# Moving the later weight tiles, and every tile allocated with them, 384 bytes further on in each partition

## The chip, the cores and the metric

The kernel runs on one core of a Trainium2 chip. The metric is the device time of one execution in microseconds. Three executions of the kernel before took 852.66, 852.87 and 853.97 us (median 852.87). An execution that was profiled took 852.58 us; its profile spans 850.8 us from the first to the last instruction.

## The reference

Three parts follow each other. The attention is banded: every query sees the 128 keys up to its own, with a bias that grows with distance. Two feed-forward layers follow, without normalisation or residual between them.

```python
scores = scale * np.matmul(q, k.transpose(0, 1, 3, 2))          # q, k, v: (4, 8, 576, 64)
mask = (rel >= 0) & (rel < window)                              # window = 128
scores = np.where(mask, scores + bias[None], -1000000000.0)
attn = softmax(scores); attn_out = np.matmul(attn, v)
x = attn_out.transpose(0, 2, 1, 3).reshape(B * S, H * D)        # (2304, 512)
h = x @ w_in;  g = h * (1.0 / (1.0 + np.exp(-1.702 * h)));  x = g @ w_out    # 512 -> 2048 -> 512
h = x @ w_in2; g = piecewise square of h, clipped at -1 and 1;  out = g @ w_out2
```

(The softmax is written out in the reference; it is shortened here.)

## The kernel before

**Attention (0 to about 138 us).** Heads are handled in 16 pairs. Queries and keys are split into a high part in fp32r (`qk_hi`) and a remainder (`k_lo`), so that a score is the sum of two fp32r matmuls with 256 columns each (L1009, the first step's L981). The probabilities are transposed on TensorE (L1022), copied, and multiplied with the values (L1043, L1037); the pair's output is transposed once more (L1052, L1057). All tiles of this stage are allocated behind `half`.

**Feed-forward (about 138 to 848 us).** Each layer is done in two phases, so there are four (u = 0 to 3). A phase has an *up* part (its quarter of x @ w_in) and a *down* part (its quarter of g @ w_out), each over three chunks c of 768 tokens. A chunk's product is a 2 x 2 block product done with seven multiplications instead of eight (P1 to P7); the seven combinations of the activations and of the weights are made by VectorE and ScalarE. Each combination is kept as a rounded fp32r value and its remainder, and a product is the sum of three fp32r matmuls for each step along the contraction: weights high x activations high, high x low, low x high. All of this is issued by `multiply` at line L1075.

**Which operand is which.** In all up parts, and in the down parts of phases 0 and 1, the weights are the stationary operand (loaded 128 x 128 by LDWEIGHTS) and the activations in `arena` are the moving one, with 384 columns. In the down parts of phases 2 and 3 ("swapped" below) it is the other way round: the stationary operand is a 128 x 128 block of `arena`, and the moving one is 256 columns of the weights.

**Where the weights lie.** Six slots hold combined weights, slot = w mod 6 for weight pair w. Slots 0 to 2 are the tile `w_first`, slots 3 to 5 the tile `w_rest`:

```python
def w_place(w):
    slot = w % W_SLOTS
    return w_first[:, slot] if slot < 3 else w_rest[:, slot - 3]
```

A phase u uses the pairs 8u to 8u+3 in its up part and 8u+4 to 8u+7 in its down part. So of the four pairs of an up part 1, 3, 2 and 1 lie in `w_rest` in phases 0 to 3. In the down parts, where the four pairs are the four steps of the contraction (in this order), the places are rest, rest, first, first (phase 0); first, first, first, rest (phase 1); first, rest, rest, rest (phase 2); rest, rest, first, first (phase 3).

**Addresses in a partition.** Tiles are allocated one behind the other. The program as compiled has 1152 bytes ahead of the first tile. `before_w_first` and `before_arena` are fillers of 64 bytes, as is `half`, of which one element is used. This gives the starts below; every slot, combination, high or low part and block inside `w_first`, `w_rest` and `arena` is a multiple of 512 bytes further on (`arena`: 1536-byte rows, so too).

| tile | start in bytes | modulo 512 | modulo 256 |
|---|---|---|---|
| `w_first` | 1216 | 192 | 192 |
| `arena` | 44288 | 256 | 0 |
| `half` | 124160 | 256 | 0 |
| `qk_hi` (attention) | 143680 | 320 | 64 |
| `w_rest` | 130368 | 320 | 64 |

The tiles of the attention and those of the feed-forward behind `half` (`d1s`, `w_rest`, `g`, `ust`, `raw_rest`) share the same memory, one set after the other. In `qk_hi` all keys and queries start at multiples of 256 bytes from the tile's start.

**Order.** Each engine's instructions are in an order written out by hand. TensorE runs P1 to P4 of a chunk and waits for `lo_made` (activations ready, from VectorE), for `seeded_b`, `seeded_c` and `d_copied` (ScalarE), and for `c21_out` and `c22_done` (the banks of earlier products read out).

Of the kernel before, what the change touches and what calls it, by code (L numbers as in the profile page):

```python
# [20 lines left out]
F32 = mybir.dt.float32  # L21
# [4 lines left out]
P = 128  # L26
# [86 lines left out]
def build(nc, qkT, v_main, v_tail, w_pairs, bias_table, identity, out):  # L113
# [3 lines left out]
    def sb(name, shape, dt, into=ctx):  # L117
        return into.enter_context(nc.sbuf_tensor(name, shape, dt))
# [17 lines left out]
    arena = sb("arena", [P, ARENA * 4 * HALF], F32R)  # L136
    raw_first = sb("raw_first", [P, 3, 4 * HALF], F32)
    wst = sb("wst", [P, 12, 2 * P], F32)
    half_line = sb("half", [P, 16], F32)
    half = half_line[:, 0:1]  # L140

    qk_raw = sb("qk_raw", [P, SPLIT_RING, WIDTH], F32, attn_ctx)
# [1914 lines left out]
```

## Time and profile before

| | |
|---|---|
| median of three runs | 852.87 us (852.66 to 853.97) |
| profiled execution | 852.58 us, of which the span 850.8 us |
| TensorE matmuls, busy | 843.7 us, 99% of the span |
| VectorE / ScalarE / GpSimd busy | 84% / 63% / 14% |
| mean granted TensorE clock | 0.999 of full |
| first and last matmul of L1075 | 138.4 us and 847.4 us |

In the timeline view a row merges neighbouring instructions of one form: start, length, engine, line, operation, output <- inputs, count. The length runs to the modelled end of the last matmul, which overlaps the next one's start. The time that TensorE needs for a matmul in a stream is therefore taken from the starts of two rows: their distance divided by the number of matmuls between them. In square brackets stands idle time before the row and what ended it.

### The profile page before, as it was taken

How to read it: one execution, taken by the hardware profiler on the slowest of the kernel's cores; microseconds unless marked ns; L12 is line 12 of the kernel's file. 1: busy time of each engine (PE TensorE's matmuls, PEld its weight loads, DVE VectorE, ACT ScalarE, POOL GpSimd, SP SyncE). 2: the span in 40 equal slices, each digit the busy share in tenths (PEclk: the TensorE clock that was granted, in tenths of full speed). 3: DMA queues.
4: the chain of work that ended last, by engine and by line, in shares of the span. 5: the costliest groups of instructions: out<-in, count | busy, mean ns of one | idle time of the engine just before them, and what ended most of it. 6: DMA issues, size and time to landing. Idle time of an engine off the chain costs nothing.

```text
span 850.8 us, 15510 instructions
## 1 busy us (share of the span) xinstructions
PE 843.7 (99%) x5744; PEld 839.7 (99%) x5744; DVE 711.4 (84%) x982; ACT 538.5 (63%) x791; POOL 116.4 (14%) x82
## 2 busy tenths in 40 slices
PE   8999999999999999999999999999999999999998
PEld 8999999999999999999999999999999999999998
DVE  7888898786988966778998987989989788889794
ACT  7778787767775546768644556767555567665441
POOL 3788988000000000000000000000000000000000
PEclk9999999999999999999999999999999999999999
DMA  8888661667676347687764772587647643888822
GB/s 203 226 213 217 191 180 67 268 253 277 250 253 226 133 150 272 250 303 240 260 246 184 287 242 105 210 282 260 235 152 262 231 154 128 291 294 304 310 83 75
DMA packets 63257, 186.45 MB, mean 219 GB/s; under 512 B 7504, under 2 KB 14352, under 8 KB 59344
## 3 DMA queue, kind: packets, MB, share of 16 engines
q1 hardware_dynamic: 62896, 185.30, 63.3%
q8 instruction: 47, 0.77, 0.3%
q14 instruction: 26, 0.21, 0.1%
q10 hardware_dynamic: 288, 0.16, 0.1%
HBM read 113.09 MB, written 72.35 MB: 218 GB/s over the span
## 4 chain that ended last, share of the span: by engine, by line
PE 92%; DVE 5%; POOL 1%; issue 1%; ACT 0%; DVEq 0%; POOLq 0%
PE ps L1075 79%; PE ps L1043 4%; PE ps L1009 3%; PE ps L1022 3%; DVE arena L1755 1%; PE ps L972 1%; POOL qk_hi L895 1%; PE ps L1037 1%; POOL k_lo L892 1%; PE ps L1052 1%; DVE probs L1645 1%; DVE qk_hi L1613 0%; DVE raw_first L1714 0%; DVE g L1787 0%; DVE raw_first L1709 0%
## 5 line engine op out<-in xcount | busy, mean ns | idle before, releaser
L1075 PE MATMUL ps<-arena,w_first 128*128 128x384 f32 x1764 | 328.6, 336 | 0.0
L1075 PEld LDWEIGHTS ps<-arena,w_first 128*128 128x128 f32 x1764 | 307.2, 188 | 0.9 <-DVE arena L1755 0.3
L1075 PE MATMUL ps<-arena,w_rest 128*128 128x384 f32 x1260 | 241.4, 336 | 0.0
L1075 PEld LDWEIGHTS ps<-arena,w_rest 128*128 128x128 f32 x1260 | 221.8, 188 | 0.6 <-issue 0.3
L1755 DVE TENSOR_TENSOR arena<-raw_first,arena 128x768 fp32r<-128x768 f32 (+1 forms) x114 | 148.8, 1318 | 75.8 <-ACT arena L1333 75.8
L1333 ACT ACTIVATE arena<-raw_first 128x768 fp32r<-128x768 f32 (+1 forms) x120 | 131.9, 1118 | 46.1 <-DVE raw_first L1714 39.7
L1075 PE MATMUL ps<-w_rest,arena 128*128 128x256 f32 x945 | 131.9, 280 | 0.6 <-DVE g L1858 0.6
L1075 PEld LDWEIGHTS ps<-w_rest,arena 128*128 128x128 f32 x945 | 120.0, 188 | 0.8 <-issue 0.8
L1075 PE MATMUL ps<-w_first,arena 128*128 128x256 f32 x567 | 85.8, 278 | 0.0
L1755 DVE TENSOR_TENSOR arena<-raw_rest,arena 128x1536 fp32r<-128x1536 f32 (+1 forms) x48 | 71.3, 1485 | 7.8 <-ACT arena L1333 7.7
L1333 ACT ACTIVATE arena<-raw_rest 128x1536 fp32r<-128x1536 f32 (+1 forms) x48 | 60.9, 1268 | 22.4 <-PE ps L1075 20.3
L1075 PEld LDWEIGHTS ps<-w_first,arena 128*128 128x128 f32 x567 | 74.8, 188 | 0.0
L1379 ACT ACTIVATE d1s<-ps 128x384 f32<-128x384 f32 (+2 forms) x72 | 35.3, 491 | 39.8 <-PE ps L1075 39.7
L1247 ACT ACTIVATE probs<-probs,neg_max 128x256 f32<-128x256 f32 (+1 forms) x128 | 54.1, 472 | 6.9 <-DVE neg_max L1645 6.9
L1043 PE MATMUL ps<-v_sb,probs_t 128*128 128x65 f32 x448 | 57.0, 268 | 0.5 <-DVE heads_out L1658 0.5
L1043 PEld LDWEIGHTS ps<-v_sb,probs_t 128*128 128x128 f32 x448 | 55.3, 191 | 0.9 <-issue 0.8
L1645 DVE CUSTOM_DVE_ANT_0 probs<-ps,bias_sb 128x256 f32<-128x256 f32 (+1 forms) x128 | 44.6, 387 | 13.3 <-PE ps L1009 8.7
L1370 ACT ACTIVATE ps<-ps 128x384 f32<-128x384 f32 (+2 forms) x72 | 34.2, 476 | 28.8 <-PE ps L1075 27.7
L1677 DVE TENSOR_TENSOR wst<-wst 128x256 f32<-128x256 f32 (+1 forms) x90 | 48.5, 539 | 2.8
L1287 ACT ACTIVATE probs_t<-ps 128x512 f32<-128x512 f32 x64 | 37.8, 590 | 18.4 <-PE ps L1022 18.1
L1009 PE MATMUL ps<-qk_hi 128*128 128x256 f32 x158 | 47.7, 324 | 1.0 <-POOL qk_hi L895 0.4
L895 POOL TENSOR_TENSOR qk_hi<-qk_raw,qk_hi 64x576 fp32r<-64x576 f32 x28 | 45.1, 1612 | 2.2
(125 smaller groups left out, 971.4 us busy)
## 6 DMA issues: line engine op xcount, KB each, us to landing
gd<-g SPq DMA_DIRECT2D x24, 1536.0 KB, 6.1
raw_rest<-gd SPq DMA_DIRECT2D x32, 768.0 KB, 5.2
wst<-w_pairs SPq DMA_DIRECT2D x32, 512.0 KB, 5.7
raw_first<-gd SPq DMA_DIRECT2D x16, 768.0 KB, 5.8
yd<-ust SPq DMA_DIRECT2D x6, 1536.0 KB, 6.3
qk_raw<-qkT SPq DMA_DIRECT2D x30, 288.0 KB, 3.8
wd<-ust SPq DMA_DIRECT2D x4, 1536.0 KB, 8.7
raw_first<-yd SPq DMA_DIRECT2D x4, 1536.0 KB, 6.7
```

Source lines behind the costliest of these rows:

```text
L895: nc.gpsimd.tensor_tensor(all_queries(qk_hi, head, LOWER), all_queries(qk_raw, head, UPPER), f32(all_queries(qk_hi, head, UPPER)), ALU.sub ...
L1009: last = nc.tensor.matmul(place, queries, k[:, key0:key0 + BAND], start=n_pass == 0 and (d > 0 or i == 0), stop=n_pass == 1 and (d > 0 or ...
L1043: last = nc.tensor.matmul(o_slot(2 * blk + e), probs_t[:, gi % 2, col:col + P], v_sb[:, h + e, max(blk - 1, 0) + piece], start=piece == 0, ...
L1075: last = nc.tensor.matmul(to, stationary, moving, start=start and n == 0, stop=n == len(steps) - 1, skip_group_check=True)
L1247: last = nc.scalar.activation(at, at, ACT.Exp, bias=neg_max[:, col:col + 1], scale=-1.0)
L1287: nc.scalar.activation(probs_t[:, gi % 2], pt_bank[gi % 2], ACT.Copy).then_inc(pt_copied[gi % 2], 1)
L1333: nc.scalar.activation(operand(k, i)[:, 0], source(k, i), ACT.Copy).then_inc(hi_made, 1)
L1370: nc.scalar.activation(b_bank(D, pos), a_bank(D, pos), ACT.Copy).then_inc(seeded_b, 1)
L1379: nc.scalar.activation(d1(D, pos), d_bank(D, pos), ACT.Copy).then_inc(d_copied, 1)
L1645: last = nc.vector.tensor_tensor_reduce(out=to[:, 0:width], in0=bank[:, i * BAND:i * BAND + width], in1=bias_sb[:, h + e, BAND - width:BAN ...
L1677: nc.vector.tensor_tensor(to, a, b, ALU.subtract).then_inc(w_added, 1)
L1755: nc.vector.tensor_tensor(at[:, 1], source(k, i), f32(at[:, 0]), ALU.subtract).then_inc(lo_made, 1)
```

## The change

The filler behind `wst` grows from 16 to 112 elements, so from 64 to 448 bytes. Everything allocated behind it starts 384 bytes later. The code of all engines, its order and all waits are the same, instruction for instruction; only addresses differ.

```diff
     raw_first = sb("raw_first", [P, 3, 4 * HALF], F32)
     wst = sb("wst", [P, 12, 2 * P], F32)
-    half_line = sb("half", [P, 16], F32)
+    half_line = sb("half", [P, 112], F32)
     half = half_line[:, 0:1]
```

After it `w_rest` starts at 130752 (192 modulo 512 and modulo 256, as `w_first`), and `qk_hi` at 144064 (192 modulo 512). `w_first`, `arena`, `raw_first`, `wst` and the start of `half` stay where they are.

## Rows read from the trace of the kernel before

**Rows 1.** The page: busy times by engine, and the chain that ended last by line.

```profile
PE 843.7 (99%) x5744; PEld 839.7 (99%) x5744; DVE 711.4 (84%) x982; ACT 538.5 (63%) x791; POOL 116.4 (14%) x82
...
PE ps L1075 79%; PE ps L1043 4%; PE ps L1009 3%; PE ps L1022 3%; DVE arena L1755 1%; PE ps L972 1%; POOL qk_hi L895 1%; PE ps L1037 1%; POOL k_lo L892 1%; PE ps L1052 1%; DVE probs L1645 1%; DVE qk_hi L1613 0%; DVE raw_first L1714 0%; DVE g L1787 0%; DVE raw_first L1709 0%
```

**Rows 2.** Groups by line and form: the matmuls of L1075 (count | busy, mean).

```profile
L1075 PE MATMUL ps<-arena,w_first 128*128 128x384 f32 x1764 | 328.6, 336 | 0.0
L1075 PE MATMUL ps<-arena,w_rest 128*128 128x384 f32 x1260 | 241.4, 336 | 0.0
L1075 PE MATMUL ps<-w_rest,arena 128*128 128x256 f32 x945 | 131.9, 280 | 0.6 <-DVE g L1858 0.6
L1075 PE MATMUL ps<-w_first,arena 128*128 128x256 f32 x567 | 85.8, 278 | 0.0
```

**Rows 3.** Timeline of PE, up parts: a long run with each tile.

```profile
201.34 15.77 PE L1075 MATMUL ps<-arena,w_first 128*128 128x384 f32 x90
216.94 1.21 PE L1075 MATMUL ps<-arena,w_rest 128*128 128x384 f32 x6
...
361.52 16.93 PE L1075 MATMUL ps<-arena,w_rest 128*128 128x384 f32 x96
378.29 1.21 PE L1075 MATMUL ps<-arena,w_first 128*128 128x384 f32 x6
```

**Rows 4.** Timeline of PE, down parts of phases 0 and 1.

```profile
238.99 1.21 PE L1075 MATMUL ps<-arena,w_rest 128*128 128x384 f32 x6
...
257.83 1.21 PE L1075 MATMUL ps<-arena,w_rest 128*128 128x384 f32 x6
...
437.34 0.68 PE L1075 MATMUL ps<-arena,w_rest 128*128 128x384 f32 x3
...
468.54 0.68 PE L1075 MATMUL ps<-arena,w_rest 128*128 128x384 f32 x3
```

**Rows 5.** Timeline of PE, swapped down parts of phases 2 and 3.

```profile
612.15 1.22 PE L1075 MATMUL ps<-w_rest,arena 128*128 128x256 f32 x9
...
639.00 1.22 PE L1075 MATMUL ps<-w_rest,arena 128*128 128x256 f32 x9
...
821.00 0.87 PE L1075 MATMUL ps<-w_rest,arena 128*128 128x256 f32 x6
...
846.08 0.87 PE L1075 MATMUL ps<-w_rest,arena 128*128 128x256 f32 x6
```

**Rows 6.** Timeline of PE, phase 3: a run's last three matmuls, and what follows.

```profile
831.81 0.50 PE L1075 MATMUL ps<-w_first,arena 128*128 128x256 f32 x3
832.15 0.87 PE L1075 MATMUL ps<-w_rest,arena 128*128 128x256 f32 x6
```

**Rows 7.** Timeline of PE, start of the program: matmuls that keep TensorE warm, scores.

```profile
6.86 2.07 PE L972 MATMUL ps<-arena 128*128 128x256 f32 x16
...
9.38 0.28 PE L1009 MATMUL ps<-k_lo,qk_hi 128*128 128x256 f32 x1
9.50 0.28 PE L1009 MATMUL ps<-qk_hi 128*128 128x256 f32 x1
```

**Rows 8.** TensorE's waits; chain in order of time; timelines of PE and of DVE.

```profile
PE ps L1075 <- DVE g L1858: 0.6, 1, 0.6
...
539.86 214.99 PE ps L1075 x1480
...
790.27 57.38 PE ps L1075 x492
...
790.27 0.92 PE L1075 MATMUL ps<-w_rest,arena 128*128 128x256 f32 x6 [0.61 <-DVE g L1858]
...
661.56 1.02 DVE L1818 TENSOR_TENSOR ust<-ps,d1s 128x512 f32<-128x512 f32 x2 [1.94 <-PE ps L1075]
```

**Rows 9.** Groups by line and form: VectorE on tiles that stay and tiles that move.

```profile
L1755 DVE TENSOR_TENSOR arena<-raw_first,arena 128x1536 fp32r<-128x1536 f32 x52 | 90.8, 1752 | 24.6 <-ACT arena L1333 24.6
L1755 DVE TENSOR_TENSOR arena<-raw_rest,arena 128x1536 fp32r<-128x1536 f32 x32 | 56.1, 1752 | 6.4 <-ACT arena L1333 6.3
```

## The prediction

> **What bounds the kernel now.** I read the page first. TensorE is busy for 99% of the span, and 79% of the chain that ended last are the matmuls of L1075 [rows 1]. So the time is the number of matmuls times what each takes in a stream, plus the few places where TensorE waits. The table of waits has a single entry in the whole feed-forward: 0.6 us on VectorE [rows 8]. The granted clock is 0.999 of full, the 2.4 GHz level, so differences between matmuls are not the clock's.
>
> The groups by form show how many matmuls use each weight tile: 1764 + 1260 with 384 columns, 567 + 945 with 256 [rows 2]. Their mean durations (336, 336; 278, 280) hardly differ, but they are lengths with a modelled end and overlap. What a matmul costs in a stream has to be read from starts in the timeline:
>
> - Up parts, only `w_first`: 216.94 - 201.34 = 15.60 us for 90 matmuls, 173.3 ns each. Only `w_rest`: 378.29 - 361.52 = 16.77 us for 96, 174.7 ns [rows 3].
> - Down part of phase 0, half `w_rest` in runs of six: 18.84 us from 238.99 to 257.83 for 9 x 12 matmuls, 174.4 ns. Phase 1, a quarter `w_rest` in runs of three: 31.20 us for 15 x 12, 173.3 ns, so no loss [rows 4].
> - Swapped down parts, phase 2 (three quarters `w_rest`): 26.85 us for 19 x 12, 117.8 ns. Phase 3 (half): 25.08 us for 18 x 12, 116.1 ns [rows 5]. At the end of a run of six with `w_first`, the last three take 832.15 - 831.81 = 0.34 us, 113.3 ns each [rows 6].
>
> The same instruction with the same shape is thus slower where the weights lie in `w_rest`, by 1.4 ns as stationary and by about 4.5 ns as moving operand. What differs is the address. My reading: a matmul streams one operand out of a partition while the next stationary operand is loaded from the same partition, and the two disturb each other unless they stand in different halves of a 256-byte stretch. `arena` starts at 0 modulo 256, `w_first` at 192 (other half: fast), `w_rest` at 64 (same half: slow).
>
> **Is it the offset, or only the tile?** `w_rest` also lies in another part of the memory, and its rows alone can't tell. The warm-up can: it takes both operands from `arena`, low in memory next to `w_first`, both at 0 modulo 256. Its 16 matmuls of 256 columns span 2.07 us; less the last one's 0.28 us, 1.79 / 15 = 119 ns [rows 7], like `w_rest` and not like `w_first`. The scores have both operands in `qk_hi` or `k_lo` (64 and 64): 9.50 - 9.38 = 0.12 us, 120 ns at that resolution [rows 7]. So same half is slow in both parts of memory. As all starts inside the tiles are multiples of 512 from the tile's, `w_rest` at 192 should behave as `w_first`.
>
> **The change part by part.** It adds and removes no instruction.
>
> 1. *Up parts.* 7 of 16 pairs lie in `w_rest`; each up part has 504 matmuls, so 7/4 x 504 = 882 matmuls save 174.7 - 173.3 = 1.36 ns: -1.2 us. Bounds: 0, if the tile and not the offset is slow, and 1.4 if the few longer intervals at changes of tile go too; I take 1.2.
> 2. *Down, phases 0 and 1.* 504 x (174.44 - 173.33) = -0.56 us, and 0.
> 3. *Down, phase 2.* 756 matmuls. With `w_first` throughout, the interval should be that of the last three of a run, 113.3: 756 x 4.46 = -3.4 us. If it were only the mean of the whole run of six (115.0, its first three at the pace of the tile before), 756 x 2.76 = -2.1 us. I take the first, since a run no longer begins behind a slow one.
> 4. *Down, phase 3.* 756 x (116.1 - 113.3) = -2.1 us on TensorE. But the chain there leaves TensorE at 754.85 (539.86 + 214.99) and returns at 790.27 [rows 8]: it runs over VectorE, and TensorE waits 0.61 us for its L1858. What TensorE saves in chunk 0, 252 x 2.8 = 0.7 us, ends in this wait, which grows to 1.3 us. Counted: 504 x 2.8 = -1.4 us (lower bound, at 115.0: -0.6).
> 5. *Attention.* All its tiles move together, from 64 to 192 modulo 256 for queries and keys: both operands change half at once and stay in the same one, so the intervals stay. Value tiles and probabilities keep their distance too. I take 0. Ends: if an operand's own offset matters, 316 score matmuls (L1009) could fall from 119 to 113.3, -1.8 us; or the attention's 1168 matmuls (5744 of the page less 4536 of L1075 and 40 others [rows 1, 2]) could each lose the 4.4 ns that separate slow from fast, +5.1 us.
> 6. *VectorE, ScalarE and the DMAs* meet the moved tiles too. L1755 takes 1752 ns on `raw_first` (stays) and 1752 ns on `raw_rest` (64 bytes past a multiple of 256) [rows 9]: 0. In phase 2 VectorE still idles 1.94 us for TensorE before L1818 [rows 8], room for the 1.1 us that a chunk gets shorter.
>
> Sum: 1.2 + 0.56 + 3.4 + 1.4 = 6.5 us (with the low values 1.2 + 0.56 + 2.1 + 0.6 = 4.4). From the profiled execution, 852.58 - 6.5 = 846.1; that lies 0.3 under the median of the runs shown, so 846.4 us.
>
> The Trainium skill speaks against all of this. Its page "TensorE: Matmul & The Clock Gate", section "Step-by-step: what each phase is for", says that loading the next tile's weights takes no SBUF read bandwidth from the running matmul, since each has a read port of its own; "SBUF — State Buffer", section "Who interferes with whom", adds that TensorE never waits for anyone there. By that rule an offset changes nothing and the time stays 852.9. The trace does not agree: one shape, one engine, one clock, and 113.3 against 117.8 ns.
>
> **The rivals.**
>
> *No effect: the slow thing is the part of memory, or the bits above 512.* The offset was read from few places, and `w_rest` keeps its place high in the memory. For it: the only fast streams in the trace use `w_first`. Against it: the warm-up, low in memory and slow. Time: 852.9.
>
> *VectorE takes it back.* It is at 84% [rows 1] and carries the chain once, from 755 to 790 us. If faster swapped parts make this recur in phase 2's chunk 0 and in all of phase 3, then only items 1 and 2 and two thirds of item 3 arrive: 1.2 + 0.56 + 2.2 = 4.0, so 848.9. For it: phase 3 is already there. Against it: a single wait in 700 us.
>
> *The attention gains too* (item 5's lower end): 846.4 - 1.8 = 844.6.
>
> *Slower.* What costs is where a tile stands by itself, and 192 is bad for the attention's streams, whose operands share one half: 1168 matmuls at +4.4 ns, while the later weights gain nothing because their slowness is that of the region. 852.9 + 5.1 = 858. It ends slower only if the attention's loss exceeds the gain behind it: against my 6.5 us it would take 5.6 ns for each of these matmuls. Against it: 119 and 120 ns in the warm-up (offset 0) and the scores (offset 64), alike.
>
> **How the numbers follow.** My forecast 0.74 (846.4; its own range 844.9 to 848.5), attention gains too 0.06, VectorE takes it back 0.09, no effect 0.07, slower 0.04. A measurement of this kernel tells about 0.2%, 1.7 us, from no change. Faster: 0.74 + 0.06 + 0.09 = 0.89; same 0.07; slower 0.04. The range takes in the attention's gain and the VectorE case: 844.5 to 849.2.
>
> **What would show it.** Starts in the timeline: `w_rest` runs in up parts at 173.3 ns; phases 2 and 3 both at 113.3 ns for all twelve matmuls of a product; the down part of phase 0 at 173.3. The wait for L1858 near 785 us grows to 1.3 us. The attention's end (first matmul of L1075 at 138.4 us) stays within 0.3 us. I am wrong if phase 2 keeps 117.8 ns (then the offset is not it), if it settles near 115 (item 3's other end), or if new waits of TensorE appear in phase 2.

## The result and the profile after

The kernel after takes 851.92 us (median of 22 runs, 849.92 to 852.60), the kernel before in the same comparison 853.32 us (22 runs, 852.48 to 853.97). The ratio is 0.998 [0.9974, 0.9986]: 1.4 us faster, or 0.16%. I had forecast 846.4 us, with 844.5 to 849.2 as the range.

Both kernels have two levels of execution time, which is needed to understand the numbers below. Of the executions after, 6 take 849.92 to 850.57 us and 16 take 851.76 to 852.60. The profiled one took 850.05 us (span 848.2), so it belongs to the lower level. Before has 10 at 852.48 to 852.95 and 12 at 853.22 to 853.97; its profiled execution (852.58) is of the lower level too. So the two profiles lie 2.5 us apart, where the medians lie 1.4 us apart.

The page after, beside [rows 1]: TensorE is still busy for 99%, and no engine does other work.

```profile
PE 841.0 (99%) x5744; PEld 836.5 (99%) x5744; DVE 711.7 (84%) x982; ACT 538.4 (63%) x791; POOL 116.5 (14%) x82
```

The groups by form after, beside [rows 2] and [rows 9]. The means are again too blunt to show the cost in a stream. VectorE's L1755 takes 1753 ns on the tile that stayed and on the tile that moved.

```profile
L1075 PE MATMUL ps<-arena,w_first 128*128 128x384 f32 x1764 | 328.4, 336 | 0.0
L1075 PE MATMUL ps<-arena,w_rest 128*128 128x384 f32 x1260 | 240.0, 336 | 0.1
L1075 PE MATMUL ps<-w_rest,arena 128*128 128x256 f32 x945 | 130.8, 280 | 0.2 <-DVE g L1858 0.2
L1075 PE MATMUL ps<-w_first,arena 128*128 128x256 f32 x567 | 86.2, 279 | 0.0
...
L1755 DVE TENSOR_TENSOR arena<-raw_first,arena 128x1536 fp32r<-128x1536 f32 x52 | 90.8, 1753 | 23.8 <-ACT arena L1333 23.5
L1755 DVE TENSOR_TENSOR arena<-raw_rest,arena 128x1536 fp32r<-128x1536 f32 x32 | 56.1, 1753 | 5.7 <-ACT arena L1333 5.7
```

TensorE's timeline after, up part of phase 1 and down part of phase 0, beside [rows 3, 4]: (377.50 - 360.86) / 96 = 173.3 ns with `w_rest`, which was 174.7, and (253.61 - 239.05) / 84 = 173.3, which was 174.4.

```profile
239.05 1.20 PE L1075 MATMUL ps<-arena,w_rest 128*128 128x384 f32 x6
...
253.61 1.20 PE L1075 MATMUL ps<-arena,w_rest 128*128 128x384 f32 x6
...
360.86 16.80 PE L1075 MATMUL ps<-arena,w_rest 128*128 128x384 f32 x96
377.50 1.20 PE L1075 MATMUL ps<-arena,w_first 128*128 128x384 f32 x6
```

TensorE's timeline after, swapped parts, beside [rows 5, 8]. Phase 2: (654.81 - 642.09) / 108 = 117.8 ns, as before. Chunk 0 of phase 3 up to 788 us also runs at 117.8 to 118. Behind the wait at 788.95 the same instructions take (823.05 - 820.33) / 24 = 113.3 ns.

```profile
642.09 1.22 PE L1075 MATMUL ps<-w_rest,arena 128*128 128x256 f32 x9
...
654.81 1.22 PE L1075 MATMUL ps<-w_rest,arena 128*128 128x256 f32 x9
...
787.18 0.87 PE L1075 MATMUL ps<-w_rest,arena 128*128 128x256 f32 x6
787.89 0.87 PE L1075 MATMUL ps<-w_first,arena 128*128 128x256 f32 x6
788.95 0.94 PE L1075 MATMUL ps<-w_rest,arena 128*128 128x256 f32 x6 [0.19 <-DVE g L1858]
789.73 0.84 PE L1075 MATMUL ps<-w_first,arena 128*128 128x256 f32 x6
790.41 0.84 PE L1075 MATMUL ps<-w_rest,arena 128*128 128x256 f32 x6
...
820.33 0.84 PE L1075 MATMUL ps<-w_rest,arena 128*128 128x256 f32 x6
...
823.05 0.84 PE L1075 MATMUL ps<-w_rest,arena 128*128 128x256 f32 x6
```

A glance at the rows' second column tells the same: six swapped matmuls are 0.87 long in the slow stream and 0.84 in the fast one.

First matmuls of the stages, read from the timelines of both profiled executions:

| stage begins | before, us | after, us | stage's own change |
|---|---|---|---|
| feed-forward, phase 0 | 138.40 | 138.59 | |
| phase 2, swapped part | 582.12 | 580.96 | -1.35 |
| phase 3, up part | 671.15 | 670.00 | +0.01 |
| phase 3, swapped, chunk 0 | 758.85 | 757.50 | -0.20 |
| chunk 1 | 788.11 | 787.18 | +0.42 |
| chunk 2 | 818.22 | 816.25 | -1.04 |
| end of L1075's starts | 847.36 | 844.70 | -0.69 |

(A row's last column is the change of the stage that ends there.) So the up parts and the unswapped down parts gave 1.35 + 0.20 us. Phase 2's swapped part gave nothing. Phase 3 gave something only behind the wait, and only in some executions, as the experiments show. Before, the wait was 0.61 us long; here it is 0.19.

### The profile page after: what moved, and what is told of

Its sections match the earlier page's. It is cut to its first block, busy times and chain, and to the rows that moved or that the text cites. A ratio compares the mean times of both kernels' runs of the same rounds, so it can differ in the third digit from the quotient of the medians.

```text
span 848.2 us, 15510 instructions
## 1 busy us (share of the span) xinstructions
PE 841.0 (99%) x5744; PEld 836.5 (99%) x5744; DVE 711.7 (84%) x982; ACT 538.4 (63%) x791; POOL 116.5 (14%) x82
## 4 chain that ended last, share of the span: by engine, by line
PE 91%; DVE 5%; POOL 1%; issue 1%; ACT 0%; DMA 0%; SPq 0%; DVEq 0%; POOLq 0%
PE ps L1075 79%; PE ps L1043 5%; PE ps L1009 3%; PE ps L1022 3%; DVE arena L1755 1%; POOL qk_hi L895 1%; PE ps L1037 1%; DVE probs L1645 1%; POOL k_lo L892 1%; PE ps L1052 1%; DVE qk_hi L1613 0%; DVE raw_first L1714 0%; DVE g L1787 0%; DMA qk_raw<-qkT 0%; DVE raw_first L1709 0%
## 5 line engine op out<-in xcount | busy, mean ns | idle before, releaser
L1075 PE MATMUL ps<-arena,w_first 128*128 128x384 f32 x1764 | 328.4, 336 | 0.0
L1075 PEld LDWEIGHTS ps<-arena,w_first 128*128 128x128 f32 x1764 | 307.3, 188 | 1.0 <-DVE arena L1755 0.6
L1075 PE MATMUL ps<-arena,w_rest 128*128 128x384 f32 x1260 | 240.0, 336 | 0.1
L1075 PEld LDWEIGHTS ps<-arena,w_rest 128*128 128x128 f32 x1260 | 220.1, 188 | 0.8 <-DVE arena L1755 0.4
L1755 DVE TENSOR_TENSOR arena<-raw_first,arena 128x768 fp32r<-128x768 f32 (+1 forms) x114 | 148.8, 1319 | 74.4 <-ACT arena L1333 74.1
L1075 PE MATMUL ps<-w_rest,arena 128*128 128x256 f32 x945 | 130.8, 280 | 0.2 <-DVE g L1858 0.2
L1075 PEld LDWEIGHTS ps<-w_rest,arena 128*128 128x128 f32 x945 | 119.5, 189 | 0.4 <-issue 0.4
L1075 PE MATMUL ps<-w_first,arena 128*128 128x256 f32 x567 | 86.2, 279 | 0.0
L1755 DVE TENSOR_TENSOR arena<-raw_rest,arena 128x1536 fp32r<-128x1536 f32 (+1 forms) x48 | 71.3, 1486 | 7.1 <-ACT arena L1333 7.0
L1075 PEld LDWEIGHTS ps<-w_first,arena 128*128 128x128 f32 x567 | 74.9, 189 | 0.0
```

Source lines behind the costliest of these rows:

```text
L1075: last = nc.tensor.matmul(to, stationary, moving, start=start and n == 0, stop=n == len(steps) - 1, skip_group_check=True)
L1755: nc.vector.tensor_tensor(at[:, 1], source(k, i), f32(at[:, 0]), ALU.subtract).then_inc(lo_made, 1)
```

## The experiments

In all of them the instructions are those of before, unless the diff says otherwise; the line of `multiply` (L1074 to L1077) shifts with the lines added ahead of it or taken out. The 95% interval of the ratio to the kernel before stands in brackets. "Distance" is the start of the weight tiles minus the start of `arena`, modulo 256 bytes: before it was 192 for `w_first` and 64 for `w_rest`, after it is 192 for both.

**The later weights alone.** The attention's tiles and `d1s` keep their places, `w_rest` moves by 384 bytes, and the tiles behind it by 512, so that their offsets modulo 512 stay.

```diff
+    sb("before_w_rest", [P, 96], F32)
     w_rest = sb("w_rest", [P, 3, OPS, 2, 2 * P], F32R)
+    sb("behind_w_rest", [P, 32], F32)
```

> Only w_rest moves by 384 bytes (with d1s ahead of it and g, ust, raw_rest behind it at their old places modulo 512, and the attention unmoved). Theory (the offset of the later weights against arena): as the changed kernel, up parts at 173.3 ns throughout (-1.9 us with the down parts of phases 0 and 1), phase 2 at 117.8 ns, about 852 us with some executions near 850. Rival (another of the moved tiles brought the gain): as before, 853.3 us, w_rest runs of the up parts at 174.7 ns.

Measured: 849.99 us (5 runs: four at 849.95 to 850.58, one at 851.92), ratio 0.997 [0.9958, 0.9982]. The timeline of PE has `w_rest` at (377.57 - 360.94) / 96 = 173.2 ns:

```profile
360.94 16.80 PE L1077 MATMUL ps<-arena,w_rest 128*128 128x384 f32 x96
377.57 1.20 PE L1077 MATMUL ps<-arena,w_first 128*128 128x384 f32 x6
```

Phase 2 stays at 117.8 ns. The kernel has the same two levels as after. With the next experiment this gives the whole effect to the offset of `w_rest`.

**The attention's tiles alone.** They move as in the change, and a second filler puts the feed-forward's tiles behind `half` back at their old place modulo 512.

```diff
-    half_line = sb("half", [P, 16], F32)
+    half_line = sb("half", [P, 112], F32)
...
+    sb("before_d1s", [P, 32], F32)
```

> Only the attention's tiles move by 384 bytes; d1s, w_rest, g, ust and raw_rest stay at their old places modulo 512. Theory: as before, 853.3 us, up parts at 174.7 ns in w_rest, first matmul of L1075 within 0.2 us of 138.4. Rival (the attention's move costs what the weights gain): 854 us or more, that matmul 0.5 us or more later.

Measured: 853.37 us (11 runs), ratio 1.0003 [0.9995, 1.0012]. The attention ends at 138.63 us. The profiled execution (853.53 us) is one of before's upper level, and its timeline shows what that level is. Behind the wait at 790.48 the intervals are (847.79 - 842.14) / 48 = 117.7 ns, where the profile of before had 116.1 [rows 5]:

```profile
790.48 0.94 PE L1076 MATMUL ps<-w_rest,arena 128*128 128x256 f32 x6 [0.61 <-DVE g L1859]
...
842.14 0.87 PE L1076 MATMUL ps<-w_first,arena 128*128 128x256 f32 x6
...
847.79 0.87 PE L1076 MATMUL ps<-w_first,arena 128*128 128x256 f32 x6
```

The 492 matmuls behind the wait times 1.6 to 1.7 ns are 0.8 us, about the distance of before's two levels. (No upper execution of before itself was profiled.)

**Is it 256 or 512 bytes?** `w_rest` at 448 modulo 512, which is again 192 modulo 256.

```diff
-    half_line = sb("half", [P, 16], F32)
+    half_line = sb("half", [P, 48], F32)
```

> The filler grows by 128 bytes in place of 384: w_rest at 192 modulo 256 as w_first, but at 448 modulo 512 where w_first is at 192. Theory (the period is 256): as the changed kernel, 850 to 852 us, up parts at 173.3 ns throughout. Rival (the period is 512): w_rest in the up parts differs from 173.3 ns, 853 us or more.

Measured: 851.97 us (11 runs: 849.99, 850.39 and nine at 851.89 to 852.57), ratio 0.9978 [0.9969, 0.9987], the levels of after. So the period is 256 bytes. The profiled execution is an upper one (851.99). Its wait is as short as after's, but the stream behind it stays at (846.24 - 842.00) / 36 = 117.8 ns:

```profile
788.92 0.95 PE L1075 MATMUL ps<-w_rest,arena 128*128 128x256 f32 x6 [0.20 <-DVE g L1858]
...
842.00 0.87 PE L1075 MATMUL ps<-w_first,arena 128*128 128x256 f32 x6
...
846.24 0.87 PE L1075 MATMUL ps<-w_first,arena 128*128 128x256 f32 x6
```

This accounts for the two levels after: 492 x (117.8 - 113.3) = 2.2 us, and the levels' usual values (849.9 and 852.0) lie 2.1 us apart. Of after itself only a lower execution was profiled; the upper one is read here, at the same distances.

**Exactly opposite halves.** All weight tiles at distance 128. This is the purest form of the mechanism on which my forecast rests. The other distances were measured in the same way, by three fillers (elements of 4 bytes):

```diff
-    sb("before_w_first", [P, 16], F32)
+    sb("before_w_first", [P, 64], F32)
...
-    sb("before_arena", [P, 16], F32)
+    sb("before_arena", [P, 32], F32)
...
-    half_line = sb("half", [P, 16], F32)
+    half_line = sb("half", [P, 32], F32)
```

> w_first and w_rest both start at 128 modulo 256, arena at 0: exactly opposite halves. Theory (the two streams disturb each other by their distance modulo 256, and at 64 or 192 they are off by a quarter, so that two intervals are possible): at 128 no disturbance, up parts 173.3 ns, swapped parts 113.3 ns in all of phases 2 and 3 and in every execution, 3.4 us less than the changed kernel's fast executions: 846.5 us. Rival (which interval holds is only a matter of the restart, at any offset): 850 to 852 us with phase 2 at 117.8 ns.

> w_first, w_rest and arena all start at 0 modulo 256. Theory (same half is slow): up parts at 174.7 ns or more in both tiles (3024 x 1.4 ns = +4.2 us on 173.3), swapped parts at 117.8 ns or more: 855.5 us or more. Rival (only the difference between the two weight tiles costs, since the stream must change its phase when the tile changes): up parts 173.3 ns, 850 to 852 us, as the changed kernel.

> w_first and w_rest both start at 64 modulo 256 (the place of w_rest before), arena at 0. Theory: up parts at 174.7 ns in both tiles (+3.3 us against 173.3 throughout in the up parts, and +0.7 to +1.4 in the down parts of phases 0 and 1), swapped parts 117.8 ns: about 856 us. Rival (only the change of tile costs): 850 to 852 us.

> w_first and w_rest both at 32 modulo 256, arena at 0. Theory (steps): as distance 0, up parts 173.3 ns, swapped 120.0 ns, 854.6 us. Rival (continuous, between 0 and 64): up parts near 174, swapped parts 118 to 119 ns, 855 us.

> w_first and w_rest both at 96 modulo 256, arena at 0. Theory (steps): as distance 64, up parts 174.6 to 176.5 ns, swapped parts 117.8 or 113.3 ns, 856 to 858 us. Rival (continuous, between 64 and 128): up parts above 175.5 ns, swapped near 118.3 ns, 858 to 860 us.

> w_first and w_rest both at 160 modulo 256, arena at 0; distance 128 gave 176.0 and 118.7 ns, with no second interval. Theory (steps): as 128, 860 us. Rival (continuous): up parts between 173.3 and 176.0, about 855 us.

> w_first and w_rest both at 224 modulo 256, arena at 0. So far, distance 0 gave 173.3 ns in the up parts and 120.0 in the swapped ones, 192 gave 173.3 and either 113.3 or 117.8. Theory (the interval is a function of the distance with steps of 64 or 128 bytes): 224 behaves as 192, 850 to 852 us. Rival (it changes continuously, so that 224 lies between 192 and 0): up parts 173.3, swapped parts a single interval between 113.3 and 120, 850 to 854 us in all executions alike.

The three sizes of the fillers are in the first column behind the distance (0 is a filler left out). Intervals are read from starts in the timelines; the last column is the ratio to before.

| distance | fillers | median, us (runs) | 384 columns, ns | swapped, 256 columns, ns | ratio |
|---|---|---|---|---|---|
| 0 | 32, 0, 64 | 854.62 (11) | 173.3 | 120.0 | 1.0011 [1.0002, 1.0019] |
| 32 | 40, 56, 8 | 851.13 (7) | 173.3 | 116.7 | 0.9973 [0.9962, 0.9984] |
| 64 | 48, 48, 16 | 856.79 (5) | 174.7, or 176.7 | 117.8, or 113.3 | 1.0036 [1.0023, 1.0048] |
| 96 | 56, 40, 24 | 856.20 (6) | 173.3; from 506 to 683 us 176.7 | 120.0 | 1.0027 [1.0016, 1.0038] |
| 128 | 64, 32, 32 | 859.99 (5) | 176.1; down parts 175.6 | 118.7 | 1.0076 [1.0064, 1.0089] |
| 160 | 8, 24, 40 | 861.37 (4) | 176.7 | 117.3, or 118.7 | 1.0091 [1.0078, 1.0104] |
| 192 (after) | 16, 16, 112 | 851.92 (22) | 173.3 | 117.8, or 113.3 | 0.998 [0.9974, 0.9986] |
| 224 | 24, 8, 56 | 857.21 (10) | 173.3, or 176.7 | 118.3 | 1.0047 [1.0033, 1.0061] |

The rows for distance 128, two stretches of the timeline of PE: (362.34 - 349.66) / 72 = 176.1 ns and (826.03 - 820.34) / 48 = 118.5 ns.

```profile
349.66 1.22 PE L1075 MATMUL ps<-arena,w_first 128*128 128x384 f32 x6
...
362.34 1.22 PE L1075 MATMUL ps<-arena,w_first 128*128 128x384 f32 x6
...
820.34 0.87 PE L1075 MATMUL ps<-w_rest,arena 128*128 128x256 f32 x6
...
826.03 0.87 PE L1075 MATMUL ps<-w_rest,arena 128*128 128x256 f32 x6
```

For distance 0, where `w_first` and `arena` stand in the same half and my mechanism wants the slowest matmuls in all parts: (826.17 - 820.41) / 48 = 120.0 ns in the swapped part, the slowest of all, but the parts with 384 columns are as fast as any.

```profile
820.41 0.88 PE L1074 MATMUL ps<-w_first,arena 128*128 128x256 f32 x6
...
826.17 0.88 PE L1074 MATMUL ps<-w_first,arena 128*128 128x256 f32 x6
```

For distance 224, two stretches of one execution with the same instruction and the same tile, 15.60 / 90 = 173.3 ns and then 12.73 / 72 = 176.8 ns. A single distance can hold more than one interval here too.

```profile
201.35 15.76 PE L1075 MATMUL ps<-arena,w_first 128*128 128x384 f32 x90
216.95 1.20 PE L1075 MATMUL ps<-arena,w_rest 128*128 128x384 f32 x6
...
349.26 1.22 PE L1075 MATMUL ps<-arena,w_first 128*128 128x384 f32 x6
...
361.99 1.22 PE L1075 MATMUL ps<-arena,w_first 128*128 128x384 f32 x6
```

For distance 160, phase 2 and then the stream behind phase 3's wait: (658.09 - 641.19) / 144 = 117.4 ns and (829.26 - 820.72) / 72 = 118.6 ns.

```profile
641.19 1.22 PE L1075 MATMUL ps<-w_rest,arena 128*128 128x256 f32 x9
...
658.09 1.22 PE L1075 MATMUL ps<-w_rest,arena 128*128 128x256 f32 x9
...
820.72 0.87 PE L1075 MATMUL ps<-w_rest,arena 128*128 128x256 f32 x6
...
829.26 0.88 PE L1075 MATMUL ps<-w_rest,arena 128*128 128x256 f32 x6
```

So two intervals at one distance are not peculiar to 192. With 256 columns they show at 64, 160 and 192, with 384 columns at 64, 96 and 224. Most changes of interval inside these executions stand beside a gap in the stream, where two starts are about 0.08 us or more further apart than usual (after has such gaps too, near 237 us for one). Not all do: at distance 96 the starts go from 176.7 to 173.3 ns apart near 683 us without any gap.

What follows: the offset decides, from 851.1 to 861.4 us with not an instruction changed, together with the draw of an interval where there are two. Opposite halves do not. The order of the distances differs for the two shapes of matmul, so there is no single "bad half".

**Distance or place?** Weights at 0 and `arena` at 64 (distance 192 as after, both places new).

```diff
-    sb("before_w_first", [P, 16], F32)
+    sb("before_w_first", [P, 32], F32)
...
-    half_line = sb("half", [P, 16], F32)
+    half_line = sb("half", [P, 48], F32)
```

> w_first and w_rest at 0 modulo 256 and arena at 64, so the distance is 192 as in the changed kernel, with other places for each. Theory (only the distance counts): up parts at 173.3 ns, swapped parts at 117.8 or 113.3, 850 to 852 us. Rival (each operand's own place in a 64- or 256-byte line counts): other intervals in one or both.

Measured: 849.98 us (5 runs: 849.42, 849.48, 849.98, 851.43, 851.58), ratio 0.9961 [0.9947, 0.9975]; 173.3 ns with 384 columns, and 117.7 ns in the swapped parts of the profiled execution (851.58 us). Two levels, as after. So at this distance the intervals do not depend on where the pair stands, and the last experiment shows the same for distance 32.

**Does a stop change the stream?** After, and before, with a stop of TensorE ahead of the swapped parts. The added wait is for TensorE's own last product, so the stream drains and starts anew.

```diff
+            if D in (24, 33):
+                pe.wait_ge(p4_done, 2 * D)
```

> The changed kernel, and TensorE waits for its own last product before the first swapped product of phase 2 and of phase 3, so its queue is empty and the stream starts anew. Theory (with all weights at one offset the swapped stream has two intervals, 113.3 and 117.8 ns, that keep themselves; a restart picks one): two stalls of 0.2 to 0.3 us, and phase 2 and phase 3 turn to 113.3 ns, -3.4 and up to -3.3 us: 847 us, perhaps only in some executions. Rival (phase 2 is slow for what other engines and the DMAs do in it): phase 2 stays at 117.8 ns, 852.4 us.

> The kernel before with the same two waits. Theory: in phase 2, where the tile changes within every product, the stream can't keep either interval for long: about 117 to 118 ns as before, so 853.3 plus 0.5 us. Rival (a restart alone is what helps, whatever the offset): phase 2 near 113.3 ns, 850 us.

Measured, after with the stops: 852.46 us (12 runs: 848.95, three at 850.53 to 850.82, eight at 852.33 to 852.97), ratio 0.9985 [0.9977, 0.9994]. In the profiled execution (848.95 us) all of phase 2 runs at (622.36 - 621.00) / 12 = 113.3 ns and so does chunk 0 of phase 3. It loses this at its next stop, the wait of 1.06 us for VectorE, and goes on at (788.07 - 786.66) / 12 = 117.5 ns:

```profile
621.00 1.18 PE L1075 MATMUL ps<-w_rest,arena 128*128 128x256 f32 x9
622.36 1.18 PE L1075 MATMUL ps<-w_rest,arena 128*128 128x256 f32 x9
...
783.97 0.84 PE L1075 MATMUL ps<-w_first,arena 128*128 128x256 f32 x6
...
785.87 0.95 PE L1075 MATMUL ps<-w_rest,arena 128*128 128x256 f32 x6 [1.06 <-DVE g L1860]
786.66 0.87 PE L1075 MATMUL ps<-w_first,arena 128*128 128x256 f32 x6
...
788.07 0.87 PE L1075 MATMUL ps<-w_first,arena 128*128 128x256 f32 x6
```

That is the forecast's phase 2, seen once: an execution with 756 matmuls at 113.3 ns is (852.4 - 848.95) = 3.4 us below the upper level of this kernel, just as item 3 has it. Chunk 0 of phase 3 was faster too, by 252 x 4.5 = 1.1 us; but that went into the wait, which grew to 1.06 us, as item 4 expected of a gain in this chunk. Before with the stops: 854.07 us (11 runs, 853.60 to 854.49), ratio 1.0011 [1.0002, 1.002]. All its swapped parts, phase 3 too, run at 117.8 ns in the profiled execution, and no execution is fast. So the stop alone is not the gain, and distance 192 alone is not either: it makes a second interval possible.

**A new draw at every stop?** After, with the wait ahead of each of the six swapped chunks.

```diff
+            if D in (24, 25, 26, 33, 34, 35):
+                pe.wait_ge(p4_done, 2 * D)
```

> The changed kernel with TensorE waiting for its own last product ahead of each of the six swapped chunks. Theory (each restart draws the interval anew, fast in about a quarter): chunks at 117.8 and at 113.3 ns side by side in one execution, and more than two levels of time between 849 and 854 us. Rival (the interval is fixed for a phase by its data, its DMAs or its place in the program): all three chunks of a phase alike, two levels.

Measured: 850.64 us (8 runs, 849.10 to 852.03, spread rather than in two levels), ratio 0.9968 [0.9958, 0.9978]. In the profiled execution (851.30 us) phase 2's chunks run at 117.8, 113.3 and 113.3 ns, phase 3's all at 117.8. The change from the first to the second chunk, (609.41 - 606.59) / 24 = 117.5 and (615.26 - 612.54) / 24 = 113.3:

```profile
606.59 0.52 PE L1075 MATMUL ps<-w_first,arena 128*128 128x256 f32 x3
...
609.41 0.52 PE L1075 MATMUL ps<-w_first,arena 128*128 128x256 f32 x3
...
612.54 0.50 PE L1075 MATMUL ps<-w_first,arena 128*128 128x256 f32 x3
...
615.26 0.50 PE L1075 MATMUL ps<-w_first,arena 128*128 128x256 f32 x3
```

So the interval is not fixed for a phase: it can change at a stop, and in all swapped streams read here it held from one stop to the next.

**Can the stream be kicked from one interval to the other?** Six extra matmuls whose moving operand stands 128 bytes further on, ahead of product 1 at the start of phase 2 and at chunk 1 of phase 3. The real product writes over their result. The second kernel has the same six without the shift.

```diff
+            if (D, n) in ((24, 0), (34, 1)):
+                other = w_op(8 * u + 4, P1).rearrange("p h n -> p (h n)")
+                for _ in range(6):
+                    nc.tensor.matmul(a_bank(D, pos)[:, 0:2 * P], operand(k, P1)[:, 0, 0, 0:P],
+                                     other[:, 32:32 + 2 * P], start=True, stop=True)
```

> The changed kernel, with six extra matmuls of 256 columns ahead of the first product of phase 2 and, in phase 3, behind TensorE's stall at chunk 1. Their moving operand starts 128 bytes further on in the weights (64 modulo 256); what they write is overwritten by the real product. Theory (the swapped stream at distance 192 keeps whichever interval it has; in the kernel before, w_first runs behind w_rest runs moved to 113.3 ns in phase 3): they bring the stream to 113.3 ns and it stays: phase 2 -3.4 us, chunks 1 and 2 of phase 3 at 113.3 in every execution, 12 extra matmuls cost 1.4 us; 848 us in most executions. Rival (only a stop and restart of the queue can change it): 851.5 to 853.5 us, phase 2 at 117.8 ns.

> The same twelve extra matmuls, with their moving operand at the place of the weights (192 modulo 256): the control. Theory: phase 2 stays at 117.8 ns, 853.3 us when phase 3 is slow, 851.3 when it is fast, as the changed kernel plus 1.4 us. Rival (any irregularity brings the fast interval): as kick_shifted, 848 us.

Measured: 853.38 us (11 runs, 853.23 to 853.93), ratio 1.0 [0.9991, 1.0009], and 853.42 us (11 runs, 853.14 to 853.84), ratio 1.0 [0.9992, 1.0009]. Both are after's upper level plus 12 x 0.118 = 1.4 us for the added matmuls. All swapped parts stay at 117.8 ns, in phase 3 behind the shifted matmuls (825.22 - 820.98) / 36:

```profile
820.98 0.87 PE L1075 MATMUL ps<-w_first,arena 128*128 128x256 f32 x6
...
825.22 0.87 PE L1075 MATMUL ps<-w_first,arena 128*128 128x256 f32 x6
```

The slow interval thus outlasts six matmuls at another distance, and the kick theory falls. One thing is left over. The six matmuls of phase 3 come first behind the wait, where after draws its interval. None of these 22 executions is in a lower level, which would be near 851.3 us, against 6 of 22 after. So what comes first behind a stop seems to matter for the draw; this was not followed up.

**A version with one level.** Distance 32 with `arena` at 64, so weights at 96.

```diff
-    sb("before_w_first", [P, 16], F32)
+    sb("before_w_first", [P, 56], F32)
...
-    sb("before_arena", [P, 16], F32)
+    sb("before_arena", [P, 56], F32)
...
-    half_line = sb("half", [P, 16], F32)
+    half_line = sb("half", [P, 8], F32)
```

> w_first and w_rest at 96 modulo 256 and arena at 64: distance 32, with other places for each than in all_at_32. Theory (only the distance counts, and at 32 there is one swapped interval): up parts 173.3 ns, swapped parts 116.7 ns in both phases, every execution within 0.7 us of 851.2. Rival (each operand's own place counts): another interval, 852 us or more, or two levels of time.

Measured: 850.63 us (7 runs, 850.52 to 851.15), ratio 0.9972 [0.9961, 0.9983]: (825.84 - 820.24) / 48 = 116.7 ns in the swapped parts of both phases, 173.3 ns elsewhere.

```profile
820.24 0.86 PE L1075 MATMUL ps<-w_rest,arena 128*128 128x256 f32 x6
...
825.84 0.86 PE L1075 MATMUL ps<-w_rest,arena 128*128 128x256 f32 x6
```

Its slowest run is below the lowest of after's upper level by 0.6 us. Against after's usual 117.8 ns it saves 1.1 ns for each of 1260 matmuls, 1.4 us; what the 252 of phase 3's chunk 0 save goes into the wait, 0.49 us here where after has 0.19. It beats before. It wasn't run beside after: its 850.63 us stand beside 852.92 of before, after's 851.92 beside 853.32, and the other kernel at distance 32 has 851.13 beside 853.55. So it is 2.3 to 2.4 us under before, after's median 1.4 and after's lower level 3.4. The two kernels with medians at 850.0 (later weights alone, `arena` at 64) have 5 runs each and hold both levels. Their medians say how often the draw was good, not that they are better than after.

## Why the prediction was wrong

The sign was right and nothing lost time where I feared it. But 6.5 us were forecast and 1.4 arrived in the median. That the time still fell is owed to items 1 and 2; the largest part of the sum, the swapped parts, gave nothing in most executions.

**Items 1 and 2 (up parts, phase 0 down) were right.** Forecast 1.2 + 0.56 = 1.8 us; the table of stages gives 1.35 + 0.20 = 1.55, and all `w_rest` runs read went to 173.3 ns. The same comes out between the levels: after's upper level lies about 1.4 us under before's upper one.

**Item 3 (phase 2) is the step that failed.** It took the last three matmuls of a `w_first` run, 113.3 ns [rows 6], for what a stream at distance 192 always takes. The warning was in my own bound: the first three of such a run were slower, and I ascribed that to the pace of the tile before. The runs show that 113.3 ns is one of two intervals which the stream can keep at distance 192, besides 117.8. After's phase 2 keeps the other. Gain 0 instead of 3.4 us, under the low end of 2.1. The prediction named this case as a sign of being wrong ("phase 2 keeps 117.8 ns"), but with the conclusion that then the offset is not it. That conclusion did not hold: the `w_rest` runs of the up parts went from 174.7 to 173.3 ns by the offset alone.

**Item 4 (phase 3) failed for the same reason.** Chunks 1 and 2 have their 113.3 ns in the profiled execution, but only 6 of 22 executions are at that level. In the others they stand at 117.8 ns, as read in the kernel whose later tiles move by 128 bytes, slower than the 116.1 of [rows 5]. Before, with its mixture of distances, phase 3 ran at 116.1 ns in one profile and at 117.7 behind the wait in another (the attention alone): the rows of before were one draw, and I read them as the property of the placement. Chunk 0 became slower, 116.1 to 117.8 ns. This cost little, as item 4's own remark on the chain says: the wait for L1858 took up 252 x 1.7 = 0.43 us of it, from 0.61 to 0.19 us. It shrank, where I had it grow to 1.3.

**Item 5 (attention, 0) was right**: 1.0003 for the attention's move alone, and its end within 0.2 us. **Item 6 was right** too: 1753 ns on either raw tile, and no new wait of TensorE in phase 2.

**The mechanism ("opposite halves are fast") fell.** Distance 128 is the second slowest of eight, and distance 0 is as fast as any with 384 columns. The 119 and 120 ns of [rows 7], both at distance 0, agree with the 120.0 ns measured there; but they are evidence for distance 0 alone, and I let them stand for every offset in the same half.

**The rivals.** "No effect: the region of memory" is refuted by the later weights alone (0.997), with every other tile at its old offset modulo 512. "VectorE takes it back" named a place where the gain would vanish, but after's chunk 0 brought no gain to it. "Slower" is refuted by the attention alone. None had the case that came: right offset, but the old interval.

The Trainium skill says on its page "TensorE: Matmul & The Clock Gate", section "Step-by-step: what each phase is for", that a weight load takes no SBUF read bandwidth from the running matmul. The runs do not agree as to time: 851.1 to 861.4 us come from the offsets of the two operands alone, with a granted clock of 0.999 or 1.0 (the 2.4 GHz level) in every run. Which part of loading or streaming the distance disturbs is not shown.

**What stays open.** The trace shows the two intervals but not what sets them. In after's trace the next weight load starts 3 to 4 ns behind a matmul's start in the fast stream and 2 to 5 ns in the slow one, so no different order of the two is seen. What decides a draw was not found, and whether distances finer than 32 bytes do better wasn't tried.

## What to carry to other kernels

When a stream of matmuls bounds the kernel, measure its interval (starts in the timeline, not mean durations) for several distances between the stationary and the moving operand modulo 256 bytes, and for each shape of matmul by itself: a filler ahead of a tile costs no time and was worth 1.2% from worst to best here. Before an interval read in one profile goes into a sum, see whether it is the same in a second execution and behind another stop. If execution times fall into levels, the interval may be a draw; a distance with one level a little above the best draw, as distance 32 here, can be the better choice.

## What the runs showed of the hardware that I had not expected

- **The interval of back-to-back fp32r matmuls depends on the distance of the operands modulo 256 bytes**: 173.3 to 176.7 ns with 384 columns, 113.3 to 120.0 ns with 256. Weights at 192 and at 448 modulo 512 behave alike, and at distances 192 and 32 moving both tiles together left the intervals as they were.
- **At some distances a stream has two intervals.** At 192 (and 64) they are 113.3 and 117.8 ns with 256 columns, or 272 and 283 cycles at the granted 2.4 GHz; at 160 they are 117.3 and 118.7; with 384 columns 173.3 and 176.7 at 96 and 224, 174.7 and 176.7 at 64. With 256 columns a stream takes one of them at a stop and keeps it for hundreds of matmuls. Levels of the execution time 2.1 us apart are the result. Phase 2 began slow in every profile at distance 192 without an added stop, and in the kernels at distance 192 without added instructions the draw behind phase 3's wait was fast in 15 of 43 executions, by their times.
- **A stop of TensorE is cheap beside that**: with the drain ahead of a chunk the two intervals around it were 340 and 222 ns in place of 118 each, so 0.33 us, while a good draw for a chunk of 252 swapped matmuls gives back 252 x 4.5 = 1.1 us.
